# Two unused pieces of memory in a conv and two-FFN kernel: where the tiles start in a partition

## The reference

```
attn: w = softmax(weight_gen) over 7 taps;  out[b, s, h, :] = sum over k of w[b, s, h, k] * x_pad[b, s + k, h, :]
x = out.reshape(8192, 192)
ffn 1: h = x @ w_in (192 x 2048);  g = max(0.01 h, h);      x = g @ w_out (2048 x 192)
ffn 2: h = x @ w_in (192 x 2048);  r = max(h, 0); g = r * r; out = g @ w_out
```

## Time and profile before

| | |
|---|---|
| median of 3 runs | 1169.27 us (1169.17 to 1169.45) |
| the profiled execution's own time | 1169.16 us |
| its span, first to last instruction | 1167.4 us |
| PE busy | 1159.9 us, 99% |
| weight loads busy (PEld) | 1118.0 us, 96% |
| DVE busy | 855.0 us, 73% |
| ACT busy | 667.4 us, 57% |

### The profile page before, as it was taken

How to read it: one execution, slowest core, us unless ns; L and a number is a source line. 1 busy time by engine, 2 the same in 40 slices (tenths; PEclk the granted TensorE clock), 3 DMA queues, 4 the chain that set the end, 5 groups by cost and what they waited for, 6 DMA issues and landing times.

```text
span 1167.4 us, 22894 instructions
## 1 busy us (share of the span) xinstructions
PE 1159.9 (99%) x10276; PEld 1118.0 (96%) x10276; DVE 855.0 (73%) x1036; ACT 667.4 (57%) x815; POOL 3.8 (0%) x11
## 2 busy tenths in 40 slices
PE   8999999999999999999999999999999999999998
PEld 6887888999999999999999999999999999999998
DVE  8888776877767786677776768777687776874574
ACT  5666656556565565655655555555555656556554
POOL 1000000000000000000000000000000000000000
PEclk9999999999999999999999999999999999999999
DMA  8211000010100101001010010100101000000000
GB/s 209 80 43 39 7 13 35 15 39 15 37 3 15 39 15 39 1 15 39 15 39 1 14 39 15 39 1 15 39 15 39 7 13 35 15 1 15 1 1 28
DMA packets 15378, 31.60 MB, mean 27 GB/s; under 512 B 1590, under 2 KB 10932, under 8 KB 15280
## 3 DMA queue, kind: packets, MB, share of 16 engines
q1 hardware_dynamic: 15280, 30.14, 8.1%
HBM read 23.84 MB, written 6.29 MB: 26 GB/s over the span
## 4 chain that ended last, share of the span: by engine, by line
PE 97%; DVE 2%; ACT 0%; issue 0%; DMA 0%; DVEq 0%
PE h_pair L958 45%; PE y_main_psum L1003 30%; PE y_rest_psum L1007 20%; PE h_pair L937 0%; DVE g_lo L733 0%; PE h_pair L923 0%; DVE g L724 0%; PE h_pair L892 0%; PE h_pair L967 0%; DMA tap_logits<-in_weight_gen_dram 0%; PE h_pair L926 0%; DVE conv_out L573 0%; PE h_pair L940 0%; PE y_main_psum L892 0%; PE y_rest_psum L885 0%
## 5 line engine op out<-in xcount | busy, mean ns | idle before, releaser
L958 PE MATMUL h_pair<-x_parts,w_in_parts 64*128 64x512 f32 x4590 | 593.0, 391 | 0.0
L958 PEld LDWEIGHTS h_pair<-x_parts,w_in_parts 64*128 64x128 f32 x4590 | 530.8, 184 | 17.5 <-issue 0.4
L1003 PE MATMUL y_main_psum<-g_hi,w_out_parts 64*128 64x512 f32 x2040 | 486.7, 394 | 1.4 <-DVE g_lo L733 1.4
L733 DVE TENSOR_TENSOR g_lo<-g,g_hi 128x1024 fp32r<-128x1024 f32 x255 | 311.7, 1222 | 152.2 <-ACT g_hi L437 87.0
L1003 PEld LDWEIGHTS y_main_psum<-g_hi,w_out_parts 64*128 64x128 f32 x2040 | 294.8, 185 | 9.3 <-DVE g_lo L733 1.8
L1007 PE MATMUL y_rest_psum<-g_lo,w_out_parts 64*128 64x512 f32 x1020 | 253.0, 391 | 0.0
L1003 PE MATMUL y_main_psum<-g_lo,w_out_parts 64*128 64x512 f32 x1020 | 252.8, 391 | 0.0
L1007 PE MATMUL y_rest_psum<-g_hi,w_out_parts 64*128 64x512 f32 x1020 | 252.8, 391 | 0.0
L425 ACT ACTIVATE g_hi<-h_pair 128x1024 fp32r<-128x1024 f32 x128 | 131.5, 1027 | 190.5 <-PE h_pair L958 190.2
L437 ACT ACTIVATE g_hi<-g 128x1024 fp32r<-128x1024 f32 x127 | 134.7, 1061 | 169.9 <-DVE g L724 169.9
L724 DVE SCALAR_TENSOR_TENSOR g<-h_pair,u 128x1024 f32<-128x1024 f32 x127 | 155.1, 1221 | 70.3 <-ACT u L431 69.8
(11 more groups left out here) (107 smaller groups left out, 476.2 us busy)
## 6 DMA issues: line engine op xcount, KB each, us to landing
x_window<-in_x_dram SPq DMA_DIRECT2D x14, 960.0 KB, 4.6
out_dram<-raw_w_in SPq DMA_DIRECT2D x16, 384.0 KB, 2.3
raw_w_out<-in_moe_w_out_dram SPq DMA_DIRECT2D x16, 192.0 KB, 3.0
tap_logits<-in_weight_gen_dram SPq DMA_DIRECT2D x16, 112.0 KB, 4.6
raw_w_in<-in_moe_w_in_dram SPq DMA_DIRECT2D x8, 192.0 KB, 3.5
raw_w_in<-in_moe_w_in_dram SPq DMA_DIRECT2D x24, 64.0 KB, 3.1
x_window<-in_x_dram SPq DMA_DIRECT2D x1, 768.0 KB
x_window<-in_x_dram SPq DMA_DIRECT2D x4, 141.8 KB
```

The source lines that it names most:

```text
L733: dve.tensor_tensor(GL[n % 4][:, :, :], gate[n % 2][:, :, :], GH[n % 4][:, :, :].bitcast(fp32), ALU.subtract).then_inc(glo_ready, 1)
L958: last = pe.matmul(h[:, i, :], w[r, slot, a, c], v[r, slot, b, :], start=first, stop=end)
L1003: return pe.matmul(ym[rows][:, :], w[r, c], g[r, i, :], start=start, stop=stop)
```

## The change

Two tiles are allocated that nothing reads or writes. No instruction is added, removed, moved or changed but for the addresses in it.

```diff
+        sb("room_for_weights", [P, 96])
+
+
 
         WI = [sb(f"w_in_parts{l}", [P, 3, 2, PR * P], fp32r) for l in range(2)]
...
         prod = [sb(f"tap_product{i}", [P, TPC * D]) for i in range(2)]
 
+        sb("room_for_inputs", [P, 32])
 
 
         X = [sb(f"x_parts{i}", [P, 3, 2, NC], fp32r) for i in range(2)]
```

## The result

The changed kernel takes 1141.24 us (median of 5 runs, 1141.16 to 1142.96) against 1169.34 us before: a ratio of 0.976, with a 95% interval of 0.975 to 0.977.

What follows compares the result with a forecast made beforehand. PE's distance from one matmul pair to the next was taken as the bound. All terms were 0: 1167.4 + 0 = 1167.4 us of span, 1169.3 us as the median, with a range of 1164.3 to 1172 us.

Steps and rivals of the forecast that it cites:

- The two paces: Pairs of matmuls on PE run at 232.2 or 233.3 ns, switching at turns; mean taken as 232.8 ns.
- these 19.5 ns: Part of each matmul pair beyond 213 ns of columns going by, 94 us over all pairs.
- the term of the weights: 9690 loads of w_in_parts and w_out_parts move from remainder 128 to 0; claimed change 0.
- the two idle pairs: Pairs on zeros at 5.72 and 5.95 us, both operands at multiples of 512, read as 0.23 us apart.
- the rival that had the sign: Weights' place has a price today: 13.6 us gained (1155.7 us) at the near end, 94 us (1075 us) far; chance 0.08.
- the 48 ns of cover: Weight loads of 184 ns stand in a distance of 232 ns, so a load could grow some 48 ns before costing anything.
- A new share of the two paces: Stretches between turns change pace: all quick 1164.3 us, chance 0.09; all slow 1174.3 us, chance 0.07.
- Alignment costs: Weight loads and moving reads at equal remainders hinder each other: up to 35 us lost, 1204 us; chance 0.04.
- inputs moved by 512: Inputs and activations move by exactly 512 bytes and keep their remainder; claimed change 0.
- turns: Operands of turn_y and turn_x loads change remainder, at most 0.4 us over 31 turns; claimed change 0.
- DVE, ACT: Convolution products and sums take 950 ns at either remainder, and PE would hide a difference; claimed change 0.
- transfers: Some targets start at other remainders; only first loads are on the chain, at worst 0.2 us either way.

Runs made afterwards that it cites:

- the sweep: Kernel before plus 14 stretches of 60 unused zero pairs at the start, weights 0 to 1536 bytes past inputs; 13.60 or 13.61 us per stretch at multiples of 256.
- only_up_matched: Kernel before with x_parts moved to 128 like the weights, g, g_hi and g_lo kept at 0, so only up steps match; 1158.78 us.
- shifted inputs: Changed kernel, in up steps of 30 of 32 segments the second half of the rows reads inputs alone 128 bytes further on; 1159.72 us.

## Why the prediction was wrong

**What bounds the kernel** was right: PE's pace from pair to pair, nothing else. The two paces, 232.2 and 233.3 ns, were read rightly too, and so was the place of the price, if there was one: "it sits in these 19.5 ns".

**The step that failed** is the term of the weights, "from 128 to 0", set to 0. It measured 28.1 us; by the starts that is 5.9 ns of the 19.5 in each pair. It rested on the two idle pairs 0.23 us apart, called "exactly what the change sets up". Their operands did match, but the starts were read to 10 ns where the question was one of 6. To the nanosecond the distance is 229 ns in one half and 235 ns in the other, 232 on average, which is the mismatched pace and not the matched one. For the pair is no sample of a settled pace: from 2.05 to 5.46 us the idle matmuls of a half start 426 to 427 ns apart, and this is the second distance after that. In the sweep such a head takes 224 to 240 ns a pair, at a perfect match, before it comes to 226.7. The text saw the rounding and the size of the sample, and still left a chance of only 0.08 to the rival that had the sign. That rival's near end, 13.6 us, was the same distance read to 230 ns, and so about half of the truth.

**The supporting rows** could not decide. Equal loads of 184 ns were taken as a sign of no price, but they stay at 184 ns while the pair gains 5.9: the price is not in the load's duration, and the 48 ns of cover are beside the point. The turns have 64 columns in a matmul instead of 512 and show no price in either place. That both paces occur over the same addresses says only that the paces are a finer matter than the match. It was never asked whether all the slow pairs have something in common, and they had: every pair of the kernel was 128 bytes off.

**The rivals.** A new share of the two paces would have given 1164.3 us; there is one pace now, and it is neither. "Alignment costs" had the right pair of streams, the load and the moving reads of one half, and the wrong sign: equal remainders are the good case. What the change asks for, multiples of 512 for both operands, is sufficient and not necessary.

**The other terms**, inputs moved by 512, turns, DVE, ACT and transfers, were right at 0, as the first two experiments show, in which all but the weights lies as in the changed kernel, or only the inputs do. The late first tokens of one profiled execution, 1.2 us, are more than the 0.2 us allowed for transfers.

By the page "TensorE: Matmul & The Clock Gate" of the Trainium skill, section "Step-by-step: what each phase is for", "Loading the next tile's weights doesn't steal SBUF read bandwidth from the running matmul." For these 32-bit operands on half the rows the measurement does not bear this out as a rule for speed: with the same load the distance between matmuls is 5.7 ns longer or not by 4 bytes of address. Whether bandwidth is what is lost no run shows. The 216 ns of its section "Back-to-back issue gap" is not reached at a match either; 226.7 ns is.

## What to carry to other kernels

Where 32-bit matmuls of 512 columns stand back to back with a weight load for each, put the stationary operand (the weights) and the moving one at starts whose difference is a multiple of 256 bytes; the place of either alone is free, and one unused tile between them does it. What counts is the load of the next weights against the reads of the running matmul, so it pays to match all steps and not one kind alone. Ask of a pace that is the same everywhere what all its instances share, before taking it as the engine's own. And take a distance between starts over a long stretch of equal pairs: one distance, read to 10 ns at the beginning of a burst, cannot bound an effect of 6 ns.

## What the runs showed of the hardware

- A pair of matmuls (64 rows each, 512 columns, 4-byte operands) at the full clock takes 226.7 ns from start to start when the place of the weights that are being loaded and that of the inputs that are being read differ by a multiple of 256 bytes, and 228.9 to 233.4 ns at the other differences tried. A difference of 4 bytes, 232.5 ns, is enough.
- Against 213 ns, the prediction's estimate for 512 columns at one a cycle, some 13 ns are left even at a match. No run here told what they are.
- How soon the quick pace is reached varies: after the first start in three to five pairs, after mismatched steps in three (`only_up_matched`) or six (shifted inputs), between stretches of zeros within one.
- The two halves of the rows keep their own pace: how far one is behind the other (3, 24 or 130 ns) does not matter for it, nor does the difference between one half's weights and the other's inputs. A slower half fell up to 0.75 us behind, about three pairs, until a turn brought them together.
- Why a pair 128 bytes off runs at two paces, 232.2 and 233.3 ns, that change at turns, is open.
